# Feed-forward blocks by pair of batches, the 64-channel parts as adjacent 64-row matmuls, four PSUM banks in turn

## The reference, cut to what matters

```
xt = x.transpose(0, 2, 1)
h = xt @ U @ V                               # U: 4224 x 32, V: 32 x 4224
u = x + h.transpose(0, 2, 1)
ch = np.maximum(u @ w_ch1, 0.0) @ w_ch2      # 192 -> 768 -> 192
return (u + ch)
```

## Time and profile before

| | |
|---|---|
| median of 3 runs | 2743.87 us (2742.2 to 2744.56) |
| the profiled execution | 2744.39 us, its span 2742.6 us |
| granted TensorE clock | 0.999 of 2.4 GHz |
| PE busy, PEld busy | 99%, 93% of the span |
| DVE, ACT, POOL busy | 78%, 38%, 7% |
| units (2253 us to the end) | 22, of 123 matmuls each, the last of 120 |

### The profile page before, as it was taken

How to read it: one execution, slowest core, us unless ns; L and a number is a source line. 1 busy time by engine, 2 the same in 40 slices (tenths; PEclk the granted TensorE clock), 3 DMA queues, 4 the chain that set the end, 5 groups by cost and what they waited for, 6 DMA issues and landing times.

```text
span 2742.6 us, 35836 instructions
## 1 busy us (share of the span) xinstructions
PE 2719.9 (99%) x14519; PEld 2558.6 (93%) x14519; DVE 2138.4 (78%) x2473; ACT 1034.2 (38%) x1392; POOL 195.4 (7%) x228
## 2 busy tenths in 40 slices
PE   8999999999999999999999999999999999999999
PEld 7898999999999999999999999999999999999999
DVE  6888977888788788888887997986767876666665
ACT  6543333333333333333333333333332443344343
POOL 0101001001011011010010010100100000000000
PEclk9999999999999999999999999999999999999999
DMA  6878769678677687696686786875962000000000
GB/s 196 203 183 217 174 194 210 155 203 198 176 201 184 178 203 179 182 219 165 191 200 165 204 189 174 199 195 166 224 156 81 35 3 29 31 29 31 29 31 35
DMA packets 102372, 412.62 MB, mean 150 GB/s; under 512 B 10656, under 2 KB 28736, under 8 KB 102080
## 3 DMA queue, kind: packets, MB, share of 16 engines
q0 software_dynamic: 31680, 151.40, 31.3%
q1 hardware_dynamic: 70528, 258.94, 26.9%
HBM read 371.37 MB, written 38.93 MB: 150 GB/s over the span
## 4 chain that ended last, share of the span: by engine, by line
PE 96%; DVE 2%; issue 1%; ACT 0%; DMA 0%; SPq 0%; DVEq 0%; ACTq 0%
PE bank L1276 24%; PE bank L1278 23%; PE bank L1277 23%; PE bank L1371 2%; PE bank L1375 2%; PE bank L1372 2%; PE bank L1374 2%; PE bank L1373 2%; PE bank L1220 2%; PE bank L1356 2%; PE bank L1359 2%; PE bank L1357 2%; PE bank L1360 1%; PE bank L1358 1%; PE bank L1325 1%; PE bank L1327 1%
## 5 line engine op out<-in xcount | busy, mean ns | idle before, releaser
L1276 PE MATMUL bank<-w_h,z_op 128*128 128x448 f32 (+1 forms) x3465 | 1234.7, 356 | 7.6 <-DVE z_op L931 2.7
L1278 PE MATMUL bank<-w_h,z_op 128*128 128x448 f32 (+1 forms) x3465 | 1228.3, 354 | 0.0
L1277 PE MATMUL bank<-w_l,z_op 128*128 128x448 f32 (+1 forms) x3465 | 1228.2, 354 | 0.0
L586 ACT ACTIVATE w_h<-w_raw 128x1344 fp32r<-128x1344 f32 (+1 forms) x385 | 485.7, 1261 | 1064.4 <-PE bank L1278 929.8
L1276 PEld LDWEIGHTS bank<-w_h,z_op 128*128 128x128 f32 x3465 | 651.9, 188 | 50.0 <-DVE z_op L931 3.0
L1278 PEld LDWEIGHTS bank<-w_h,z_op 128*128 128x128 f32 x3465 | 651.8, 188 | 40.9
L1277 PEld LDWEIGHTS bank<-w_l,z_op 128*128 128x128 f32 x3465 | 652.1, 188 | 39.8
L943 DVE TENSOR_TENSOR w_l<-w_raw,w_h 128x1344 fp32r<-128x1344 f32 (+1 forms) x385 | 567.7, 1475 | 63.0 <-ACT w_h L586 62.2
L561 POOL DMA_DIRECT2D w_raw<-in_w_tok x220 | 192.8, 898 | 1866.7 <-DVE w_l L943 1127.0
L1153 DVE SCALAR_TENSOR_TENSOR hid_l<-bank,hid_h 128x384 fp32r<-128x384 f32 x264 | 144.4, 557 | 153.0 <-ACT hid_h L811 149.7
L979 DVE TENSOR_TENSOR Y<-Y,bank 128x1344 f32<-128x1344 f32 (+1 forms) x105 | 154.7, 1473 | 103.0 <-PE bank L1278 102.3
(11 more groups left out here) (132 smaller groups left out, 2956.6 us busy)
## 6 DMA issues: line engine op xcount, KB each, us to landing
w_raw<-in_w_tok SPq DMA_DIRECT2D x220, 672.0 KB, 4.5
w_raw<-in_w_tok POOLq DMA_DIRECT2D x220, 672.0 KB, 6.8
z_raw<-z_out SPq DMA_DIRECT2D x85, 576.0 KB, 6.7
z_out<-zf SPq DMA_DIRECT2D x65, 384.0 KB, 6.5
x_win<-in_xin SPq DMA_DIRECT2D x22, 585.0 KB, 5.9
out<-res SPq DMA_DIRECT2D x22, 576.0 KB, 3.0
v_raw<-in_v SPq DMA_DIRECT2D x11, 144.0 KB, 3.2
w_raw<-in_w SPq DMA_DIRECT2D x1, 1536.0 KB, 7.1
```

The lines of the kernel that those rows point to most:

```text
L586: nc.scalar.activation(w_h[:, s % WRING, :, 0:n], w_raw[:, SLOT[s], :, 0:n], ACT.Copy).then_inc(wh_ready, 1)
L1276: mm(to, zh, wh, start=(k == 0 and not goes_on), stop=False, skip_group_check=goes_on)
L1277: mm(to, zh, wl, start=False, stop=False, skip_group_check=goes_on)
L1278: last = mm(to, zl, wh, start=False, stop=(k == KC - 1), skip_group_check=goes_on)
```

## The change

The blocks of a unit are made in pairs: `up(ff)` makes block `ff` of both batches at once, in two banks, and `f` now goes even, odd, even, odd. For the tile of its own each batch keeps its three 128-row matmuls. The shared tile is split like the others into a high and a low part (`u2_h`, `u2_l`), and its products are three for each batch, each of **64 rows**, one batch in partitions 0 to 63 and the other in 64 to 127, taken in turn: six matmuls. `half_s`, the repeated and zero-filled weight blocks and their preparation go away. The ring has four banks. On PE the order is up(0), up(1), down(0), down(1), up(2), down(2), down(3) and so on. `low_rank` stands as three matmuls in a row ahead of up(3). Both batches are finished at a unit's end. The inputs of the next unit are split by one instruction on ACT and one on DVE (1152 elements each) instead of three and three. `down` waits for `res_ready` before it first writes a result bank.

```diff
-G_BANK = (6, 3)
-
-
-def ring_use(f, last):
-
-    return f if last else f + min(max(f - FT + 1, 0), TP)
+G_BANK = (6, 5)
...
+LOW_RANK_AT = 3
+U_BANKS = 4
+
+
+def use_of(i, p, f, last):
+    return (PAIRS * i + p) * RING + f + (TP if f >= 2 * LOW_RANK_AT and not last else 0)
+
+
+def low_rank_use(i, p, t):
+    return (PAIRS * i + p) * RING + 2 * LOW_RANK_AT + t
...
@@ scalar, unit_act @@
-                    if f == 7:
-                        move(0)
-                    if f == 8 and not last:
-                        u2_whole_hi(i, at(i, 2 * RING, RING * p + TP + FT + 2 * TP - 1), 1 - p, nxt)
-                    if f == 9 and not last:
-                        for odd in range(2):
-                            u2_half_hi(i, 1 - p, odd, nxt)
-                move(1)
+                    if f == 2 * LOW_RANK_AT + 1 and not last:
+                        u2_hi_of(TP + low_rank_use(i, p, TP), 1 - p, nxt)
+                for odd in range(2):
+                    move(odd)
...
@@ vector, unit_dve @@
-                    dve.wait_ge(hid_free, at(i, 2 * HID, HID * p + FT * (odd + 1) + 4))
+                    dve.wait_ge(hid_free, at(i, 2 * HID, HID * p + HID - 1 + odd))
...
-                    if f == FT + 1:
-                        finish_whole(0)
-                    if f == FT + 2:
-                        finish_half(0)
...
-                finish_whole(1)
-                finish_half(1)
+                    if f == 2 * LOW_RANK_AT + 3 and not last:
+                        u2_lo_of(2 * i + p + 1, 1 - p, nxt)
+                for odd in range(2):
+                    finish_whole(odd)
+                    finish_half(odd)
...
@@ tensor, unit_pe @@
-                def up(f):
-
-                    odd, ff = divmod(f, FT)
-                    use = ring_use(f, last_unit)
-                    pe.wait_ge(bank_out, at(i, 2 * RING, RING * p + use + 1))
+                def up(ff):
                     cols = slice(ff * P, (ff + 1) * P)
-                    o = bank[use % 3][:, 0:GW]
-                    mm(o, w1_h[:, odd, cols], full_h[:, p, odd], start=True, stop=False)
-                    mm(o, w1_h[:, odd, cols], full_l[:, p, odd], start=False, stop=False)
-                    mm(o, w1_l[:, odd, cols], full_h[:, p, odd], start=False, stop=False)
-                    mm(o, w1_h[:, 2 + odd, cols], half_s[p][:, odd], start=False, stop=False)
-                    mm(o, w1_l[:, 2 + odd, cols], half_s[p][:, odd], start=False, stop=True).then_inc(f1_ready, 1)
+                    uses = [use_of(i, p, 2 * ff + odd, last_unit) for odd in range(2)]
+                    sums = [bank[use % U_BANKS][:, 0:GW] for use in uses]
+                    uh, ul = u2_h[:, p], u2_l[:, p]
+
+                    def free(odd):
+                        if uses[odd] >= U_BANKS:
+                            pe.wait_ge(bank_out, TP + uses[odd] - U_BANKS + 1)
+
+                    def whole(odd, end):
+                        mm(sums[odd], w1_h[:, odd, cols], uh[:, 2 * odd], start=not end, stop=False)
+                        mm(sums[odd], w1_h[:, odd, cols], ul[:, 2 * odd], start=False, stop=False)
+                        return mm(sums[odd], w1_l[:, odd, cols], uh[:, 2 * odd], start=False, stop=end)
+
+                    free(0)
+                    whole(0, False)
+                    free(1)
+                    rows = (slice(0, 64), slice(64, P))
+                    for odd in range(2):
+                        mm(sums[odd], w1_h[rows[odd], 2, cols], uh[rows[odd], 1], start=(odd == 1), stop=False)
+                    for odd in range(2):
+                        mm(sums[odd], w1_h[rows[odd], 2, cols], ul[rows[odd], 1], start=False, stop=False)
+                    for odd in range(2):
+                        end = mm(sums[odd], w1_l[rows[odd], 2, cols], uh[rows[odd], 1], start=False, stop=(odd == 0))
+                        if odd == 0:
+                            end.then_inc(f1_ready, 1)
+                    whole(1, True).then_inc(f1_ready, 1)
...
+                    if first and (i or p):
+                        pe.wait_ge(res_ready, 4 * (PAIRS * i + p) - 2 + 2 * odd)
...
+                for ff in range(FT):
+                    if ff == LOW_RANK_AT and not last_unit:
+                        pe.wait_ge(vs_l, i + p + 1)
+                        for t in range(TP):
+                            use = low_rank_use(i, p, t)
+                            pe.wait_ge(bank_out, TP + use - U_BANKS + 1)
+                            low_rank(1 - p, t, use % U_BANKS)
+                    up(ff)
...
+                    if ff:
+                        down(2 * ff - 2)
+                        down(2 * ff - 1)
```

More of the change, by code:

```diff
@@ L316, in build @@
         with ExitStack() as first:
-            half_0 = sb(first, "half_0", [P, 2, GW], F32R)
+            sb(first, "to_g_parts", [P, 2 * GW])
             g_parts = sb(first, "g_parts", [2 * RANK, GW])
@@ L568, in _ @@
             pool.wait_ge(acc_free, done)
[L569 removed]
+            for n, zero in enumerate((w2_y[:, 0, :, 64:P], w2_y[:, 1, :, 0:64])):
                 if n:
@@ L745, in late_copy @@
                 else:
-                    b = 1 if n == 7 else 3
-                    nc.scalar.activation(w1_h[:, b], w1_raw[:, b], ACT.Copy).then_inc(late_hi, 1)
+                    nc.scalar.activation(w1_h[:, 1], w1_raw[:, 1], ACT.Copy).then_inc(late_hi, 1)
             def v_hi(i, n):
@@ L754, in v_hi, with u2_hi_of @@
                 nc.scalar.activation(v_s[:], v_raw[:], ACT.Copy).then_inc(vs_h, 1)
-            def u2_whole_hi(i, added, p, cols):
+            def u2_hi_of(added, p, cols):
                 act.wait_ge(bank_out, added)
[L759 to L764, removed]
+                nc.scalar.activation(u2_h[:, p], Y[:, TP * p:TP * (p + 1), cols], ACT.Copy).then_inc(u2_hi, 1)
             def copy_g(p):
@@ L803, in move @@
                     src, dst = (slice(64, P), slice(0, 64)) if not odd else (slice(0, 64), slice(64, P))
-                    act.wait_ge(hid_free, at(i, 2 * HID, HID * p + FT * (odd + 1) + 4))
+                    act.wait_ge(hid_free, at(i, 2 * HID, HID * p + HID - 1 + odd))
                     nc.scalar.activation(moved[dst], bank[5 + 2 * odd][src, 0:GW], ACT.Copy).then_inc(moved_ready, 1)
-                nxt = bass.ds(at(i, GW, GW * p), GW)
+                nxt = slice(GW * (i + p), GW * (i + p + 1))
                 for f in range(HID):
                     act.wait_ge(f1_ready, at(i, 2 * HID, HID * p + f + 1))
-                    act.wait_ge(hid_free, at(i, 2 * HID, HID * p + f + 1))
-                    nc.scalar.activation(hid_h[:, f % 4], bank[ring_use(f, last) % 3][:, 0:GW],
+                    if not first or f >= 4:
+                        act.wait_ge(hid_free, at(i, 2 * HID, HID * p + f - 3))
+                    nc.scalar.activation(hid_h[:, f % 4], bank[use_of(i, p, f, last) % U_BANKS][:, 0:GW],
                                          ACT.Relu).then_inc(relu_hi, 1)
-                    if first and f == 3:
+                    if first and f == 1:
                         split_g(1)
-                    if f == 7:
-                        move(0)
-                    if f == 8 and not last:
-                        u2_whole_hi(i, at(i, 2 * RING, RING * p + TP + FT + 2 * TP - 1), 1 - p, nxt)
-                    if f == 9 and not last:
-                        for odd in range(2):
-                            u2_half_hi(i, 1 - p, odd, nxt)
-                move(1)
+                    if f == 2 * LOW_RANK_AT + 1 and not last:
+                        u2_hi_of(TP + low_rank_use(i, p, TP), 1 - p, nxt)
+                for odd in range(2):
+                    move(odd)
             copy_g(1)
@@ L1071, in w1_lo @@
             def w1_lo(b):
[L1072 to L1075, removed]
+                dve.wait_ge(late_hi, (1, 8, 2)[b])
+                vec.tensor_tensor(w1_l[:, b], w1_raw[:, b], w1_h[:, b].bitcast(F32), ALU.subtract).then_inc(w1_split, 1)
             def v_lo(i, n):
@@ L1086, in add_low_rank, with u2_lo_of @@
                 vec.tensor_tensor(y, bank[b][:, 0:GW], y, ALU.add).then_inc(bank_out, 1)
[L1088 to L1097, removed]
+            def u2_lo_of(n, p, cols):
+                dve.wait_ge(u2_hi, n + 1)
+                vec.tensor_tensor(u2_l[:, p], Y[:, TP * p:TP * (p + 1), cols], u2_h[:, p].bitcast(F32),
                                   ALU.subtract).then_inc(u2_lo, 1)
@@ L1174, in finish_half @@
                     vec.tensor_tensor(half, half, moved[rows], ALU.add).then_inc(res_ready, 1)
-                nxt = bass.ds(at(i, GW, GW * p), GW)
+                nxt = slice(GW * (i + p), GW * (i + p + 1))
                 for f in range(HID):
-                    if FT <= f < FT + TP and not last:
-                        add_low_rank(i, p + 1, 1 - p, f - FT, (ring_use(f, last) - 1) % 3, nxt)
+                    if f == 2 * LOW_RANK_AT and not last:
+                        for t in range(TP):
```

(11 more changed lines are left out.)

72 lines of the change are left out of this document (26 added, 46 removed).

## The result

| | before | after |
|---|---|---|
| median | 2744.21 us (4 runs) | 2767.31 us (2767.03 to 2768.01, 4 runs) |
| ratio | | 1.0086, 95% interval 1.0074 to 1.0097 |
| profiled execution, its span | 2744.39, 2742.6 us | 2767.24, 2765.4 us |
| first matmul of the units to the start of the last one | 2253.82 to 2737.14: 483.3 us | 2253.72 to 2759.30: 505.6 us |
| last matmul's start to the end of the span | 5.5 us | 6.1 us |

A forecast was written before the change was run, and what follows sets the result against it. PE's matmul stream was taken as the bound: 2744.39 + 52.9 (64-row stretches) - 7.2 (unit starts) + 0.9 (end) = 2791.0, less 0.5 to the median: 2790.5 us, 1.7% slower; range 2765 to 2840 us, chance 0.80.

The forecast's parts named there:

- the first rival, parallel loads: 64-row stretches: both halves load at once, pairs cost a slot, +0.218 us at 132 places; 2768 us, chance 0.20.
- The slot and PE as the bound: Whole kernel: PE is 96% of the chain; a 384-column matmul takes a 0.176 us slot, 123 slots a unit.
- Going into 64 rows and back, 0.394 us: Around each 64-row stretch: each change empties the array (0.09 us) and exposes one load (0.107 us), 0.394 both ways.
- The loads inside, 0.711 us: Six 64-row matmuls of a stretch: weight loads follow each other, 5 x 0.107 + 0.176 = 0.711 us.
- the bounds: Streams of six 64-row matmuls: three slots (0.528 us) if pairs run side by side, six (1.056 us) without overlap.
- The unit starts, -7.2 us: First down of a unit: 21 waits for DVE vanish, as PE needs relu_lo(0) only after two longer ups; -7.2 us.
- the rival's +2 us for starts with `v_lo`: Unit starts under parallel loads: shorter ups leave 10 starts with `v_lo` waiting 0.11 + 0.107 us, about +2 us.
- Other edits: Low-rank additions just covered, banks and splits hidden; DVE's two finishes in one chain at the program's end, +0.9 us.
- No overlap: 64-row matmuls stream one after the other, +0.746 us at 132 places; 2836 us, chance 0.15.
- no switch: Row changes cost nothing: pairs at one slot 2730 us, chance 0.13; loads in a row 2740 us, chance 0.07.

The follow-up runs named there:

- `short_columns`: Changed kernel with 128 instead of 384 moving columns in the 64-row matmuls, and two DVE steps moved behind the next unit's relu_lo: 2732.18 us, 0.9959 of before.
- `dve_order`: Kernel before with only DVE's order changed: last add of the odd batch's half behind the next unit's relu_lo(0), v_lo behind relu_lo(2): 2736.18 us, ratio 0.9972.
- `order_128`: Changed kernel's order, but with the 128-row halves of the kernel before, ten slots for a block pair: 2741.20 us, ratio to before 0.9992.
- the first experiment: The run `three_then_three`: changed kernel with its 64-row matmuls reordered; 2767.19 us.
- `three_then_three`: Changed kernel with a block pair's six 64-row matmuls as three of one half, then three of the other: 2767.19 us, ratio to before 1.0086.
- `six_then_six`: Changed kernel with every 64-row matmul made twice, six of the lower half and then six of the upper: 2897.54 us, ratio to before 1.0562.

## Why the prediction was right or wrong

The time was within the range and the direction right; the forecast of 2790.5 us was 23 us too high, twice the change that was measured, and what happened is the first rival, parallel loads, at 2768 us. The range held because it took in that rival, not because the forecast's own mechanism did.

- *The slot and PE as the bound*: right. The full slots of the changed kernel are 0.176 us as before.
- *Going into 64 rows and back, 0.394 us*: right. The trace after has the same 0.09 us and the same bare load each way, and three numbers of stretches give 0.40 each. That this price, read from fp32 matmuls of 96 weight columns, would carry over was argued and not known then. This is the term that made the kernel slower: 132 x 0.394 = 52.0 us, against 132 x 0.176 = 23.2 us that the pairs save.
- *The loads inside, 0.711 us*: the step that failed. "If loads follow each other, as in all rows of before" was the wrong end: the stretch's inside is 0.528 us, three slots. 132 x 0.183 = 24.2 us, the whole miss of 23.2 and 1 us more. The rows on which it rested had one half in use, so they could say that half the rows don't load faster, but not whether two halves load at once. The choice between the bounds was made "as it rests on measured loads"; what had been measured was one load, not two. The rule of the Trainium skill (TensorEngine Tiling (Array Packing), Tiling Modes, Key Properties) that different tiles load and multiply in parallel was set aside for want of a row; `short_columns` bears it out with a pair of loads every 0.11 us.
- *The unit starts, -7.2 us*: right in the changed kernel, where no start waits. `dve_order` got 6.8 us by taking away the same waits and nothing else. The timing within was 0.2 us off for two finishes in a row. That is why the rival's +2 us for starts with `v_lo` didn't come (its 2768 was in part luck), and it showed in `order_128`.
- *Other edits*: the low-rank addition is just covered, as said. The end cost 0.7 us, forecast 0.9.
- *No overlap* (2836) and *no switch* (2730, 2740) are out: starts in pairs, and a gap of 0.09 us at each change, in the trace after.
- The idea that matmuls must be neighbours to run in pairs, which the first experiment took for granted, was wrong.

Left open: whether the look-ahead is counted in matmuls or in instructions, loads included. Longer stretches with all of the reference computed were not tried: over three blocks they need six sums beside four result banks, more than the eight banks that the kernel uses, and over two blocks all four banks of the ring at once, whose cost in waits no run shows. The changed kernel with DVE's order of `dve_order` has no waits left to lose, so it was not run either.

## What to carry to other kernels

Splitting a matmul of short contraction into pairs of row halves makes two matmuls cost one slot, and each visit to that mode costs 0.40 us here, 2.3 slots of 384 columns: it pays only where a visit replaces at least three such slots more than it uses, so gather them into few long stretches, if the sums leave room for it, or stay with padded 128-row matmuls. A small wait that shows as no idle time in PE's matmuls can be found by start-to-start times over a slot, and moving two instructions of another engine took 7 us of them away. Where a price is read from one unit in use, it doesn't say what two units at once cost; keep both ends equally likely until a row shows two.

## What the runs showed of the hardware

- TensorE started matmuls of a free row half ahead of up to three matmuls of the busy half that stood before them in the program (`three_then_three`: no loss; `six_then_six`: 2897.5 against 2835.6 us for the same twelve in turn). The Trainium skill (TensorE: Matmul & The Clock Gate, Part 3: Packing small matmuls, The mechanism) says that matmuls start and end in program order; here the trace differs for different row halves. A semaphore on the last matmul of one half may then be no proof that the other half's earlier ones are done (not tried: in these kernels each half signals for itself).
- At a change between 128 and 64 rows TensorE starts nothing for 0.09 us behind the end of the slot, and the next load is bare (0.107 us for 128 weight columns): 0.40 us for a change there and back, for the fp32r matmuls of the units, and the same 0.09 us around the fp32 ones of L1312.
- Weight loads of two row halves run at the same time: a pair of loads every 0.11 us (`short_columns`), where one 64-row load alone takes 0.1 us (`six_then_six`).
- A wait for DVE ahead of a weight load cost the matmul stream its length and the bare load behind it (before: the next matmul follows 0.28 instead of 0.176 us later; 7.2 us for 21 waits, and `dve_order` got 6.8 back).
